# Three of four Fourier transforms moved into attention slots, u kept where x lies, and the first MLP block's x prepared in the last slot

## The reference

```
q, k, v: (4, 8, 576, 64)   w_phi: (64, 128)   w1: (512, 2048)   w2: (2048, 512)

phi(x) = [exp(p - m), exp(-(p - m))],  p = x @ w_phi,  m = max|p| of the row
kv, z  = sum_s phi(k)^T v,  sum_s phi(k)
attn   = (phi(q) @ kv) / (phi(q) @ z + 1e-6)              # per batch and head
x      = attn, heads side by side                          # (4, 576, 512)
u      = x + real(fft(fft(x, axis=1), axis=2))
y      = u + relu(norm(u) @ w1) @ w2                       # norm: mean 0, variance 1
out    = y + relu(norm(y) * g @ w1b) @ w2b                 # a second pair of weights
```

## Time and profile before

| | us |
|---|---|
| median of 3 runs | 1125.23 |
| lowest, highest | 1124.24, 1131.91 |
| profiled execution | 1124.07 |
| its span (first to last instruction) | 1122.2 |
| PE busy in the span | 1075.2 (96%) |
| DVE, ACT, POOL busy | 693.0, 527.7, 369.9 |
| mean granted clock of PE, as a share of the full one | 0.988 |

### The profile page before, as it was taken

The page is one execution under the profiler, slowest core; times in us unless marked ns, Lnnn a source line. Parts: engine busy times, 40 slices in busy tenths (PEclk is TensorE's granted clock), DMA queues, the critical chain, the costliest instruction groups (busy, mean ns, idle before and its releaser), DMA issues.

```text
span 1122.2 us, 18062 instructions
## 1 busy us (share of the span) xinstructions
PE 1075.2 (96%) x6296; PEld 967.6 (86%) x6296; DVE 693.0 (62%) x1213; ACT 527.7 (47%) x945; POOL 369.9 (33%) x355
## 2 busy tenths in 40 slices
...
GB/s 127 65 63 63 63 63 63 42 81 49 85 40 134 39 75 58 75 57 75 75 46 68 75 48 66 68 64 57 76 57 83 106 75 38 76 131 61 54 19 57
DMA packets 73176, 76.31 MB, mean 68 GB/s; under 512 B 24595, under 2 KB 53909, under 8 KB 73109
## 3 DMA queue, kind: packets, MB, share of 16 engines
...
...
## 4 chain that ended last, share of the span: by engine, by line
PE 81%; DVE 6%; ACT 4%; issue 3%; POOL 3%; DMA 1%; SPq 1%; DVEq 0%; ACTq 0%; POOLq 0%
PE bank L898 31%; PE bank L877 26%; PE bank L370 7%; PE bank L354 5%; PE bank L314 4%; PE bank L334 3%; PE bank L591 2%; DVE w1op L1046 2%; DVE stats L1116 1%; ACT xraw L952 1%; PE bank L841 1%; PE bank L624 1%; SPq L788 1%; DMA rawqk<-qkT 1%; POOL x_sums L994 1%
## 5 line engine op out<-in xcount | busy, mean ns | idle before, releaser
L898 PE MATMUL bank<-w2op,hid 128*128 128x512 f32 x1728 | 429.8, 393 | 0.0
L898 PEld LDWEIGHTS bank<-w2op,hid 128*128 128x128 f32 x1728 | 321.9, 188 | 58.6
L877 PE MATMUL bank<-x_T,w1op 128*128 128x384 f32 x1152 | 222.1, 341 | 13.3 <-issue 6.1
L877 PEld LDWEIGHTS bank<-x_T,w1op 128*128 128x128 f32 x1152 | 207.7, 191 | 23.5 <-issue 15.2
L877 PE MATMUL bank<-x_B,w1op 128*128 128x384 f32 x864 | 177.9, 347 | 18.7 <-DVE part_s L1081 8.8
L877 PEld LDWEIGHTS bank<-x_B,w1op 128*128 128x128 f32 x864 | 152.6, 191 | 33.2 <-issue 28.5
L1013 POOL TENSOR_TENSOR w_sums<-st_w 128x256 f32<-128x256 f32 x48 | 39.4, 820 | 383.5 <-DVE w1op L1046 383.5
L1101 DVE SCALAR_TENSOR_TENSOR hid<-part_s,hid 128x384 fp32r<-128x384 f32 x144 | 121.5, 867 | 49.6 <-ACT hid L1097 47.3
L1097 ACT ACTIVATE hid<-part_s 128x384 fp32r<-128x384 f32 x144 | 74.7, 525 | 156.9 <-DVE part_s L1081 154.5
L1060 DVE TENSOR_TENSOR w2op<-st_w,w2op 128x1024 fp32r<-128x1024 f32 x48 | 66.4, 1383 | 120.5 <-ACT w2op L1056 120.5
L1046 DVE TENSOR_TENSOR w1op<-w_sums,w1op 128x1024 fp32r<-128x1024 f32 x48 | 68.1, 1419 | 75.2 <-ACT w1op L1041 75.2
...
## 6 DMA issues: line engine op xcount, KB each, us to landing
st_w<-w1a SPq DMA_DIRECT2D x24, 512.0 KB, 3.4
st_w<-w2a SPq DMA_DIRECT2D x24, 512.0 KB, 3.6
st_w<-w1b SPq DMA_DIRECT2D x24, 512.0 KB, 3.3
st_w<-w2b SPq DMA_DIRECT2D x24, 512.0 KB, 3.6
...
```

What stands on the lines that cost most here:

```text
L877: last = nc.tensor.matmul(dst, w1op[g % 2][:, a, W1OP.index(w), c, :], xop[x][:, b, c, :], start=name in ("M2", "M1", "M7") and k_ == 0, s ...
L898: last = nc.tensor.matmul(acc[t0 + t][:, :], hid[name, g % 2][:, x, P * t:P * (t + 1)], w2op[g % 2][:, y, j, :], start=first and k_ == 0, ...
```

## The change

**Transforms in slots.** The loops over pairs are written out, and each engine has a function for a slot (`pe_slot`, `act_slot`, `dve_slot`, `pool_slot`). Batch b = 0, 1, 2 is folded in slot 4b + 5, goes through stage A in slot 4b + 6, stage B in slot 4b + 7, and is mixed into u in slot 4b + 8. Batch 3 is transformed after the last slot (16, which only finishes pair 15), as before.

**PSUM.** The projections of a pair are five units (0, 1: q; 2: the rest of both; 3, 4: k) that take three banks in turn; the transforms have two banks (6 and 7), so that each output waits until the one before the last is taken; batch 3 also uses banks that attention has left.

**Order in a slot.** Unit 3 and unit 4 now stand between products with v, the first products with v stand behind T1, and the last ones ahead of unit 4. ACT's splitting of the next pair stands behind the first copy instead of the second.

**u in place.** `ubuf` and `sp_relay` go. x lies in `xall[batch][column]`; u is mixed there, and the MLP and the stores to `out` use its tiles. Only the last 64 rows of each batch are packed to `tails` by 8 DMAs (`sp_pack`). The blocks of the MLP are now formed of the 16 full tiles and two tiles of tails.

**x of block 0.** Statistics of its tiles 0 to 3 are taken after slot 11 and of 4, 5 after slot 15; the tiles are normalised, transposed and copied in slot 16, POOL's sums of them stand ahead of the last add and the folds of batch 3. w1 of steps 0 and 1 is loaded in slot 4, its sums for step 0 are made after slot 14. The MLP's functions are otherwise as before, but for banks (products in banks 5 and 7), places in memory and the conditions that guard them.

```diff
+    def batch_in(g, k):
+        b, r = divmod(g - 4 - k, 4)
+        return b if r == 0 and 0 <= b < B - 1 else None
+
+    def pe_slot(pe, g):
+        l = g - 1
+        a_, b_ = batch_in(g, 2), batch_in(g, 3)
...
+        if l >= 0:
+            pe_transpose(pe, l, 0)
+        if g != 1 and g < PAIRS:
+            for u in range(3):
+                pe_unit(pe, g, u)
+        if l >= 0:
+            pe_transpose(pe, l, 1)
+            pe_kv(pe, l, 0)
+            pe_transpose(pe, l, 2)
+            pe_kv(pe, l, 1)
+        if g < PAIRS:
+            pe_unit(pe, g, 3)
+        else:
+            pe_xT(pe, 0, 0)
+            pe_xT(pe, 0, 1)
+        if l >= 0:
+            pe_transpose(pe, l, 3)
+            pe_kv(pe, l, 2)
+        if g < PAIRS:
+            pe_unit(pe, g, 4)
+        if l >= 0:
+            pe_transpose(pe, l, 4)
+        if g == PAIRS:
+            pe_xT(pe, 0, 2)
+            pe_xT(pe, 0, 3)
+        if a_ is not None:
+            pe_stepA(pe, a_, "S0")
+            pe_stepA(pe, a_, "S1")
+        if b_ is not None:
+            pe_stepB(pe, b_, "Q0")
+            pe_stepB(pe, b_, "Q1")
+        if l >= 0:
+            pe_num(pe, l, 0)
+        if g == PAIRS:
+            pe_xT(pe, 0, 4)
...
+        if l >= 0:
+            pe_num(pe, l, 1)
+        if g == PAIRS:
+            pe_xT(pe, 0, 5)
+        if a_ is not None:
+            pe_stepA(pe, a_, "CX")
+        if b_ is not None:
+            pe_stepB(pe, b_, "P1")
+            pe_stepB(pe, b_, "P2")
+
+    def dve_slot(dve, g):
+        f_, a_, b_, m_ = (batch_in(g, k) for k in (1, 2, 3, 4))
+        if g >= 2:
+            for a in range(2):
+                dve_finish(dve, g - 2, a)
+        if m_ is not None:
+            dve_sumdiff(dve, m_, 2)
+        if g < PAIRS:
+            dve_features(dve, g, 0)
+        if f_ is not None:
+            dve_diff(dve, f_)
+            dve_fold_odd(dve, f_)
+        if a_ is not None:
+            dve_fold_lo(dve, a_, True)
+            dve_fold_lo(dve, a_, False)
+        if m_ is not None and g < PAIRS:
+            dve_mix(dve, m_)
+        if g < PAIRS:
+            dve_features(dve, g, 1)
...
+        if b_ is not None:
+            dve_sumdiff(dve, b_, 0)
+            dve_sumdiff(dve, b_, 1)
...
+    def act_slot(act, g):
...
+        if l >= 0:
+            act_q_copy_out(act, l, 0)
+        if g + 1 < PAIRS:
+            act_split_qk(act, g + 1)
+        if a_ is not None:
+            act_fold_hi(act, a_, True)
+        if l >= 0:
+            act_q_copy_out(act, l, 1)
...
             sp.dma_start(gcol[:, :], g_dram).then_inc(s_gain, 16)
-            with sp.Fori(1, PAIRS - 1) as g:
-                sp_qk(sp, g + 1)
+            for g in range(1, PAIRS):
+                if g + 1 < PAIRS:
+                    sp_qk(sp, g + 1)
                 sp_v(sp, g)
+                if g == 4:
+                    sp_w1(sp, 0)
+                    sp_w1(sp, 1)
...
+            for g in range(3, PAIRS):
+                dve_slot(dve, g)
+                if g == 11:
+                    dve_ln_stats(dve, 0, range(4))
+                if g == 15:
+                    dve_ln_stats(dve, 0, range(4, BT))
+            dve_slot(dve, PAIRS)
             dve_ln_rstd(dve, 0)
             dve_xn(dve, 0, 0)
             dve_xn(dve, 0, 1)
-            dve_mix_G(dve, B - 2)
+            dve_mix(dve, B - 2)
             dve_xn(dve, 0, 2)
             dve_xn(dve, 0, 3)
...
+            dve_w1_lo(dve, 0, 1)
+            dve_w1_lo(dve, 0, 2)
+            dve_xn(dve, 0, 4)
+            dve_xn(dve, 0, 5)
+            for a in range(2):
+                dve_finish(dve, PAIRS - 1, a)
```

More of the change, by code:

```diff
@@ new lines, in program @@
+    o = ATT
+    w1op[0], o = at("w1op0", [P, 2, 7, KH, P], F32R, o)
+    tf, o = at("x_sums", [P, 4, KH, TOK], F32, o)
+    assert o <= early_end
+    for n in XOP:
+        xop[n], o = at(f"x_{n}", [P, 2, KH, TOK], F32R, o)
+    assert o <= DFT + 256, o - DFT
+    o = DFT + 256
+    w1op[1], o = at("w1op1", [P, 2, 7, KH, P], F32R, o)
+    st2[0], o = at("st_w2_0", [P, 2, DM], F32, o)
+    for n in TMPS:
+        tmp[n], o = at(f"part_{n}", [P, TOK], F32, o)
+    assert o <= folded_end
+    for n in BLOCKS:
+        hid[n, 0], o = at(f"hid{n}_0", [P, 2, TOK], F32R, o)
@@ new lines, in pe_stepA @@
+    def pe_stepA(pe, b, name):
+        if name == "S0":
+            pe.wait_ge(oo_hi, b + 1)
+            pe.wait_ge(oo_lo, b + 1)
+            pe.wait_ge(s_zero, 4)
+        if name == "C0":
+            pe.wait_ge(ee_hi, 2 * b + 2)
+            pe.wait_ge(ee_lo, 2 * b + 2)
+        dft_bank_free(pe, b, name)
+        src, mat = (oo, "ss") if name[0] == "S" else (ee, "cs")
+        c0, c1 = {"0": (0, P), "1": (P, 2 * P), "X": (HD, HD + 1)}[name[1]]
+        dst = dft_bank(b, name)[0:c1 - c0, 0:HS if name[0] == "S" else NS]
+        steps = [(src[x][0:ROWS[t], t, c0:c1], cst[mat, y][0:ROWS[t], t, :]) for t in range(HT) for x, y in HL_]
+        if mat == "cs":
+            steps += [(ex[x][0:1, c0:c1], cst["odd", "hi"][0:1, :]) for x in ("hi", "lo")]
+        for k_, (lhsT, rhs) in enumerate(steps):
+            last = nc.tensor.matmul(dst, lhsT, rhs, start=k_ == 0, stop=k_ == len(steps) - 1)
+        last.then_inc(a_done, 1)
@@ new lines, in pe_stepB @@
+    def pe_stepB(pe, b, name):
+        if name == "Q0":
+            pe.wait_ge(t_lo, len(A_OUT) * b + 2)
+            pe.wait_ge(t_hi, len(A_OUT) * b + 2)
+        if name == "P0":
+            pe.wait_ge(t_lo, len(A_OUT) * (b + 1))
+            pe.wait_ge(t_hi, len(A_OUT) * (b + 1))
+        dft_bank_free(pe, b, name)
+        c0 = P * int(name[1])
+        c1 = c0 + ROWS[int(name[1])] + (name == "P2")
+        src, mat = (tsn, "sd") if name[0] == "Q" else (tc_, "cd")
+        steps = [(src[x][:, t, c0:c1], cst[mat, y][:, t, :]) for t in range(2) for x, y in HL_]
+        if mat == "cd":
+            steps += [(tx[x][0:1, c0:c1], cst["alt", "hi"][0:1, :]) for x in ("hi", "lo")]
+        dst = dft_bank(b, name)[0:c1 - c0, 0:NK]
+        for k_, (lhsT, rhs) in enumerate(steps):
+            last = nc.tensor.matmul(dst, lhsT, rhs, start=k_ == 0, stop=k_ == len(steps) - 1)
+        last.then_inc(b_done, 1)
@@ new lines, in dve_slot @@
+    def dve_slot(dve, g):
[17 more added lines that the diff above has]
+            dve_features(dve, g, 1)
+        if f_ is not None:
+            dve_fold_even(dve, f_)
+        if a_ is not None:
+            for name in A_OUT:
+                t_split(dve, a_, name, False)
+        if b_ is not None:
+            dve_sumdiff(dve, b_, 0)
+            dve_sumdiff(dve, b_, 1)
+        if m_ is not None and g < PAIRS:
+            dve_mix_G(dve, m_)
@@ L1118, in dve_ln_stats @@
         need(dve, sd_done, i)
-        for t in range(BT):
+        for t in tiles:
             dve.wait_ge(st_done, BT * i + t + 1)
@@ L1349, in _ @@
-            act_attention(act, 0, range(1, PPI))
+            act_const_hi(act, "ss")
+            act_slot(act, 1)
             for n in ("cd", "sd", "odd", "alt"):
-                nc.scalar.copy(cst[n, "hi"][:], raw[n][:]).then_inc(s_split_hi, 1)
-            with act.Fori(1, ITERS - 1) as i:
-                act_attention(act, i)
-            act_attention(act, ITERS - 1, split=False)
-            act_attention(act, ITERS, range(1), ahead=False)
-            act_fold_hi(act, 0, True)
-            act_ex_ends(act, 0)
```

854 lines of the change are left out of this document (398 added, 456 removed).

## The result

The changed kernel takes 1161.81 us, the median of 4 runs (1158.86 to 1166.99), the kernel before on the same chip 1125.62: 1.0315 times as long, 95% interval 1.0259 to 1.0371. The profiled execution took 1166.99 us; its span is 1165.2 us and its mean granted clock 0.957, against 1122.2 and 0.988 before. It is the slowest of the four; the others have 0.961, 0.965 and 0.966.

A forecast was written before the change was run, and what follows sets the result against it. PE was taken to bound the sequence up to 304.10, leaving 18 idle us and a slow clock after it to win. Terms 2.5 + 5.0 + 2.15 + 1.2 + 3.9 - 1.8 = +12.95 on 1124.07 gave 1137.0 us, range 1123 to 1149.

The forecast's parts named there:

- Slots without a transform: Slots 2, 3, 4, 5, 8, 9, 12, 13: PE waits 0.62 us for ACT's copy of T4 before the numerators, +5.0 us.
- Transforms in slots: Transforms of batches 0 to 2 add 43.74 us to full slots and take it off after them; nothing won as such.
- Slot 1: ACT's split waits for its load ahead of the second copy, so PE's third transposes wait: +2.5 us.
- Slot 5: Two w1 loads queue ahead of pair 6's q and k; the delayed split costs PE 1.2 us, between 0 and 3.4.
- Slot 12: Statistics of four x tiles on DVE delay a division and a projection unit: 2.15 us together, between 0 and 4.
- The tail: Last slot's first transposes to first MLP step's last product: 67.6 us, PE idle 16 before stage A; net +3.9 us.
- half of the 3.7 us that PE ran back to back at the lower clock: Last stages A and B: slow clock after the idle time adds 1.85 us to their 14.58.
- u in place: Dropping 32 DMAs that laid u out anew removes one ACT wait in MLP step 1: -1.8 us.
- the first (PE makes up its waits): In the slots, weight loads running ahead swallow short waits; +2.1 us is left, 1126 us; chance 0.15.
- the short tail: In the tail, DVE and POOL stop colliding (3.5 us) and stage A has no slow clock (1.85): 1131.6 us; chance 0.2.
- The collisions of the third: Slots 5, 9, 13, 6, 10, 14: DVE waits for POOL, 1.6 us each, delaying PE; 9.6 us, 1146.6; chance 0.2.
- the four cases: Whole kernel: forecast 1137 us (chance 0.45) and three rivals at 1126 (0.15), 1131.6 (0.2) and 1146.6 (0.2).

## Why the prediction was wrong

It said 1137.0 us, and 1123 to 1149; 1161.8 were measured. Slower was right and the steps were the right ones, but one term was missing. Against the profiled execution 30.0 us are short, and they are found as follows.

- *Slots without a transform.* 14.70 us, with the 0.46 us wait for the copy of T4 in all eight. Priced at +0.62, measured +0.78: 1.3 us short in all. Right.
- *Transforms in slots.* 22.48 and 20.06 us in slots 10 and 11, 42.54 together for 42.40 worked out. Right. Slot 14 takes 2.6 us more and slot 15 1.9, both by the clock.
- *Slot 1.* Priced +2.5, and it waits 1.93 us where it was said to. But the clock falls within that wait and is at 0.50 from 24 to 31: 2.6 us short.
- *Slot 5.* Priced +1.2, the wait is 1.50. The slot grew by 9.7 us, slot 6 by 1.2 beyond slot 10: 9.7 short. This is the largest miss, on the smallest term.
- *Slot 12.* Waits of 0.70 and 0.82 us, 1.99 us in all (16.69 less 14.70) for 2.15. Right; no fall behind them.
- *The tail.* The 16 us on PE ahead of the last stage A were 16.66, and 33 to 35 us from there to the last product were 40.7 (341.12 to 381.86). From T0 of the last slot the sum had 67.6 us and the trace has 80.8. The last slot's own work lasts to 23.4 and not 17.4, with the clock at 0.50 for 14 of these us; stages A and B take 23.54 and not 16.4. The step that failed reads "half of the 3.7 us that PE ran back to back at the lower clock": I took the time that the clock needs to recover from one place of the trace before, and the lower level lasted for 20.6 us of unbroken work here. The term had 1.85 us, it measured 9.0 (23.54 less 14.58).
- *u in place.* -1.8 priced; the stretch from M3 of step 0 to M2 of step 2 went from 20.6 to 18.4 us, -2.2, and the rest of the MLP is 1.0 shorter. Right.

Nearly all of the 30 us is the granted clock: 8.2 in slot 5, 1.2 in slot 6, 2.6 in slot 1, 4.5 in slots 14 and 15, about 5.5 in the last slot, 7.1 in the last stages beyond what I had allowed. The fault in the prediction has one sentence: waits were priced at their own length. It fails first in the step on slot 5, "I give the split a delay that costs PE 1.2 us": the wait was 1.50 us and the two slots cost 10.9. What makes the clock fall in slot 14, 4.5 of the 30 us in the profiled execution, stays open but for the order of the products. Of the rivals, the first (PE makes up its waits) is refuted by the 0.46 us rows; the short tail did not come. The collisions of the third are there, but none reaches PE: no wait of PE in slots 5, 6, 9, 10, 13 and 14 is for DVE. DVE's rows in slot 5, the first while POOL folds, the second behind it:

```profile
92.66 2.48 DVE L618 TENSOR_TENSOR oo_raw<-OL,OH 128x765 f32<-128x765 f32 x1 [4.78 <-POOL OL L593]
...
99.62 0.94 DVE L629 TENSOR_TENSOR ee_raw<-EL,EH 128x765 f32<-128x765 f32 x1
```

Operations of the same size take 2.48 and 0.94 us; the first takes 2.50 and 2.52 in slots 9 and 13. None of the four cases had the clock outside the tail, though the earlier trace rows had shown 0.50 after an idle time, and the range ended 10 us short of the fastest run.

The Trainium skill (TensorE: Matmul & The Clock Gate, "Terms") puts the price of a throttled stretch at the throttled time times one less the ratio, that is half of it. Slots 5 and 6 agree: 20 us at 0.50 with PE busy in 19.54, and 9.4 us lost. The same page of the Trainium skill ("HAM oscillation — how this bites in real kernels") tells of waits for data, of 3 to 5 us, behind which the work begins at the lower level. The rows at 87 to 103 in the kernel before with waits of 3.42 us agree; the row at 88.27 shows that here a wait of 1.50 us was enough, with the fall 0.6 us behind it.
